# Softmax reciprocals widened by ScalarE and turned in whole transposes, and a reordered opening, in a fused attention and gated feed-forward kernel

## What is computed

```python
q_rot, k_rot = rotate(q), rotate(k)
scores = np.matmul(q_rot, k_rot.transpose(0, 1, 3, 2)) / sqrt(64)
attn = np.exp(scores - scores.max(axis=-1, keepdims=True))
attn = attn / (attn.sum(axis=-1, keepdims=True) + 1e-9)
x = np.matmul(attn, v)                       # to (2304, 512)
h = x @ w_in
g = np.maximum(h, 0) + alpha * np.minimum(h, 0)
out = g @ w_out
```

## Time and profile before

| | us |
|---|---|
| median of 3 runs (666.73 to 667.43) | 666.87 |
| the profiled execution | 668.44 |
| its span | 666.6 |
| PE busy in the span | 654.8 |
| DVE, ACT, POOL busy | 338.9, 320.5, 266.9 |
| attention, from the start to the first feed-forward matmul | 253 |

### The profile page before, as it was taken

How to read it: one execution, slowest core, us unless ns; L and a number is a source line. 1 busy time by engine, 2 the same in 40 slices (tenths; PEclk the granted TensorE clock), 3 DMA queues, 4 the chain that set the end, 5 groups by cost and what they waited for, 6 DMA issues and landing times.

```text
span 666.6 us, 14994 instructions
## 1 busy us (share of the span) xinstructions
PE 654.8 (98%) x5566; PEld 562.1 (84%) x5566; DVE 338.9 (51%) x779; ACT 320.5 (48%) x730; POOL 266.9 (40%) x254
## 2 busy tenths in 40 slices
PE   7899999999999999999999999999999999999998
PEld 6687778778877777988899999999999999999996
DVE  4677887878888773455523332333233323332222
ACT  2688888887888885333332223222322232223223
POOL 3755788888766223222222222222222222222222
PEclk8999999999999999999999999999999999999999
DMA  5596455544544436000010001000100010001001
GB/s 142 133 240 183 106 122 135 124 108 112 121 113 110 92 104 253 1 0 1 1 49 0 1 0 48 1 1 0 47 0 0 0 47 0 0 0 48 1 0 48
DMA packets 73309, 41.58 MB, mean 62 GB/s; under 512 B 59812, under 2 KB 64292, under 8 KB 72740
## 3 DMA queue, kind: packets, MB, share of 16 engines
q1 hardware_dynamic: 72978, 40.62, 23.3%
q10 hardware_dynamic: 274, 0.16, 0.1%
HBM read 22.95 MB, written 4.72 MB: 41 GB/s over the span
## 4 chain that ended last, share of the span: by engine, by line
PE 96%; DVE 1%; ACT 1%; DMA 1%; SPq 0%; issue 0%; POOL 0%; DVEq 0%
PE banks L772 30%; PE banks L801 30%; PE banks L713 9%; PE banks L607 8%; PE banks L687 5%; PE banks L636 3%; PE banks L709 3%; PE banks L581 2%; PE banks L658 2%; PE banks L663 1%; PE banks L562 1%; DMA cos_sb<-in_cos 1%; PE banks L589 1%; PE banks L666 0%; PE banks L654 0%
## 5 line engine op out<-in xcount | busy, mean ns | idle before, releaser
L529 POOL TENSOR_TENSOR g_lo<-g,g_hi 128x384 fp32r<-128x384 f32 (+1 forms) x98 | 99.7, 1018 | 306.9 <-ACT g_hi L959 303.7
L1123 DVE TENSOR_SCALAR g<-banks,alpha_sb 128x384 f32<-128x384 f32 (+1 forms) x98 | 59.7, 610 | 249.2 <-ACT pos L950 249.2
L772 PE MATMUL banks<-x_hi,w_in_lo 128*128 128x384 f32 x384 | 129.3, 337 | 0.0
L772 PE MATMUL banks<-x_hi,w_in_hi 128*128 128x384 f32 x384 | 129.2, 337 | 0.0
L772 PE MATMUL banks<-x_lo,w_in_hi 128*128 128x384 f32 x384 | 129.0, 336 | 0.0
L950 ACT ACTIVATE pos<-banks 128x384 f32<-128x384 f32 x96 | 47.2, 491 | 169.2 <-PE banks L772 169.2
L801 PE MATMUL banks<-w_out_hi,g_hi 128*128 128x512 f32 x288 | 114.9, 399 | 0.3
L801 PE MATMUL banks<-w_out_hi,g_lo 128*128 128x512 f32 x288 | 112.9, 392 | 0.0
L801 PE MATMUL banks<-w_out_lo,g_hi 128*128 128x512 f32 x288 | 111.9, 389 | 0.0
L959 ACT ACTIVATE g_hi<-g 128x384 fp32r<-128x384 f32 (+1 forms) x98 | 50.9, 519 | 116.5 <-DVE g L1126 116.5
L844 ACT ACTIVATE prob<-prob,nmax 128x576 f32<-128x576 f32 x128 | 98.3, 773 | 1.7 <-DVE prob L1014 1.7
(11 more groups left out here) (80 smaller groups left out, 920.4 us busy)
## 6 DMA issues: line engine op xcount, KB each, us to landing
q_swap<-q_nat SPq DMA_DIRECT2D x32, 256.0 KB, 3.6
k_swap<-k_nat SPq DMA_DIRECT2D x32, 144.0 KB, 3.1
out<-stage SPq DMA_DIRECT2D x18, 256.0 KB, 2.0
raw_q<-in_q SPq DMA_DIRECT2D x32, 128.0 KB, 2.8
raw_k<-in_k SPq DMA_DIRECT2D x32, 128.0 KB, 2.5
raw_v<-in_v SPq DMA_DIRECT2D x32, 128.0 KB, 2.3
w_in_raw<-in_moe_w_in SPq DMA_DIRECT2D x4, 1024.0 KB, 6.0
w_out_raw<-in_moe_w_out SPq DMA_DIRECT2D x8, 512.0 KB, 6.6
```

The costliest lines, as they stand in the source:

```text
L529: nc.gpsimd.tensor_tensor(g_lo[f % 2][:, part], g[f % 2][:, part], g_hi[f % 2][:, part].bitcast(F32), ALU.subtract).then_inc(g_lo_done, 1)
L772: mm = nc.tensor.matmul(h_ps[f % 2], w[:, j, cols], xx[:, j, :], start=(step == 0), stop=(step == 3 * CT - 1))
L1123: nc.vector.tensor_scalar(g[f % 2][:, part], h_ps[f % 2][:, part], 0.0, alpha_sb[:, f:f + 1], ALU.min, ALU.mult).then_inc(neg_done, 1)
```

## The change

The reciprocals: ACT widens them first (`widen`), copying each of the eight columns of the tiles 64 times into `inv_wide` (128 x 512, SBUF). PE then makes four whole 128 x 128 transposes of it in place of eight matmuls. DVE, no longer ACT, copies the 512 columns to `inv_sb`. The sums are kept in rows of three with a gap (`rsum` 3 x 4) and read as 3 x 3, the 1e-9 is an immediate of a `tensor_scalar` in place of a second operand, and the reciprocal follows at once.

The opening: ACT issues the keys and their remainders, SP the rest, so the cosines and the identity move up in SP's queue. U_MIXED is turned ahead of U_K in the work before pair 0, and in pair 0 it lies in the keys' bank pair (bank 2) in place of bank 1.

```diff
-OPENING_BANK = {U_Q: 2, U_K: 3, U_MIXED: 1}
+OPENING_BANK = {U_Q: 2, U_K: 3, U_MIXED: 2}
...
+        if u == U_K and isinstance(p, int) and p == 0:
+            return U_MIXED
...
-            rsum = sb(att, "rsum", [P, 2, TILES])
+            rsum = sb(att, "rsum", [P, 2, 3, 4])
+            sums = sb(att, "sums", [P, TILES])
...
-            load(0, 0)
+            heads(sp, 0, 0)
+            joined(sp, 0, 0)
             table(sp, cos_sb, cos, cos_in)
-            load(0, 1)
             sp.dma_start(ident[:, :], eye).then_inc(ident_in, 16)
...
             table(act, sin_sb, sin, sin_in)
+            joined(act, 0, 1)
+            heads(act, 0, 1)
...
-                if u != U_KQREM and has_prev(p):
+                if u == U_INV:
+                    pe.wait_ge(wide_done, p)
+                elif u == U_MIXED and has_prev(p):
                     pe.wait_ge(inv_done, p)
...
                     for i in range(QT):
-                        for r, n in zip(HEADS, (A_TILES[i], B_TILES[i])):
-                            mm = nc.tensor.matmul(bank[r, i * P:(i + 1) * P], inv[:, par, n:n + 1].to_broadcast([P, D]),
-                                                  ident[:, :], start=True, stop=True)
+                        mm = nc.tensor.transpose(bank[:, i * P:(i + 1) * P],
+                                                 inv_wide[:, i, :, :].rearrange("p h d -> p (h d)"), ident[:, :])
...
             turn(-1, -1, U_Q)
+            spread(-1, -1, U_MIXED)
             run_in(4)
             turn(-1, -1, U_K)
-            spread(-1, -1, U_MIXED)
             run_in(6)
...
+            def widen(p, t):
+                if not has_prev(p):
+                    return
+                act.wait_ge(inv_done, p)
+                if not (isinstance(p, int) and p == 1):
+                    act.wait_ge(turned, unit_count(p - 1, U_INV))
+                nc.scalar.activation(inv_wide[:, :, :, :], inv[:, (t - 1) % 2, 1:].rearrange("p (h i) -> p i h", h=2)
+                                     .unsqueeze(3).to_broadcast([P, QT, 2, D]), ACT.Copy).then_inc(wide_done, 1)
...
                 p = b * PAIRS + t
+                widen(p, t)
                 flat(p, U_QREM, t)
...
-                flat(p, U_INV, t)
                 flat(p, U_PA[0], t)
...
-                    nc.vector.tensor_tensor(rsum[:, par, :], rsum[:, par, :], tiny[:, :].to_broadcast([P, TILES]),
-                                            ALU.add).then_inc(sum_done, 1)
+                    nc.vector.tensor_scalar(sums[:, :], rsum[:, par, :, 0:3], 1e-9, None, ALU.add).then_inc(sum_done, 1)
...
-                    nc.vector.reciprocal(inv[:, par, :], rsum[:, par, :]).then_inc(inv_done, 1)
+                    nc.vector.reciprocal(inv[:, par, :], sums[:, :]).then_inc(inv_done, 1)
...
+                if h == 0:
+                    u = U_INV
+                    dve.wait_ge(turned, unit_count(p, u))
+                    nc.vector.tensor_copy(inv_sb[:, 0:QT * P], t_ps[bank_of(p, u)]).then_inc(evac[bank_of(p, u)], 1)
+                    dve.wait_ge(evac[bank_of(p, u)], evac_count(p, u))
                 dve.wait_ge(pv_done, n + 1)
...
                 reciprocals(p, t, 0)
+                reciprocals(p, t, 1)
                 flat(p, U_KQREM, t)
                 maxima(p, t, REM_TILE)
-                reciprocals(p, t, 1)
```

More of the change, by code:

```diff
@@ L95, in bank_of, with rank @@
         return OPENING_BANK.get(u, BANK_OF[u]) if isinstance(p, int) and p == 0 else BANK_OF[u]
+    def rank(p, u):
+        return U_Q + 0.5 if p < 0 and u == U_MIXED else u
     def tally(p, u, counted):
         if isinstance(p, int):
-            return sum(exists(r, w) for r in range(-1, p + 1) for w in counted if r < p or w <= u)
+            return sum(exists(r, w) for r in range(-1, p + 1) for w in counted
+                       if r < p or rank(p, w) <= rank(p, u))
         return p * len(counted) + (tally(PAIRS, u, counted) - PAIRS * len(counted))
@@ L194, in build @@
             raw_v = [sb(att, f"raw_v{i}", [P, ST, P]) for i in range(2)]
[L195 removed]
+            inv_wide = sb(att, "inv_wide", [P, QT, 2, D])
+            assert 2 * ST + QT >= CT * MT
             until_prob = used[0]
@@ L281, in build @@
         inv_done = sem("inv_done")
+        wide_done = sem("wide_done")
         pv_done = sem("pv_done")
@@ L340, in table, with heads, joined @@
             eng.dma_start(dst[:, QT, :], src[0:REM, QT, :].unsqueeze(0).to_broadcast([2, REM, D])).then_inc(landed, 16)
+        def heads(eng, p, side):
+            src, raw, landed = ((q_h, raw_q, q_in), (k_h, raw_k, k_in))[side]
+            for h in range(2):
+                eng.dma_start(raw[:, 0:QT, h * D:(h + 1) * D],
+                              src[p * 2 + h, 0:QT * P, :].rearrange("(t p) d -> p t d", p=P)).then_inc(landed, 16)
+        def joined(eng, p, side):
+            eng.dma_start(raw_q[side * REM:(side + 1) * REM, QT, :].rearrange("p (h d) -> p h d", h=2),
+                          (q_h, k_h)[side][bass.ds(p * 2, 2), QT * P:S, :].rearrange("h p d -> p h d")
+                          ).then_inc(q_in, 16)
         HEADS = (slice(0, D), slice(D, P))
@@ L358, in load @@
                     sp.wait_ge(rope_step, (p - 1) * 8 + side * 4 + 3)
-                for h in range(2):
-                    sp.dma_start(raw[:, 0:QT, h * D:(h + 1) * D],
-                                 src[p * 2 + h, 0:QT * P, :].rearrange("(t p) d -> p t d", p=P)).then_inc(landed, 16)
+                heads(sp, p, side)
                 if side == 0:
-                    for i, rems in enumerate((q_h, k_h)):
-                        sp.dma_start(raw_q[i * REM:(i + 1) * REM, QT, :].rearrange("p (h d) -> p h d", h=2),
-                                     rems[bass.ds(p * 2, 2), QT * P:S, :].rearrange("h p d -> p h d")).then_inc(landed, 16)
+                    for i in range(2):
+                        joined(sp, p, i)
             def swap(p, par, side):
@@ L646, in spread @@
                 elif u != U_INV and has_next(p):
-                    turned_in(p, 1)
-                if u != U_KQREM and has_prev(p):
+                    turned_in(p, 0 if isinstance(p, int) and p < 0 else 1)
+                if u == U_INV:
+                    pe.wait_ge(wide_done, p)
+                elif u == U_MIXED and has_prev(p):
                     pe.wait_ge(inv_done, p)
@@ L881, in flat @@
                     jobs = [(pt_half(t % 2, u), half_bank(bank))]
-                else:
-                    if not (isinstance(p, int) and p == 1):
-                        act.wait_ge(x_done, (p - 1) * 2)
-                    jobs = [(inv_sb[:, 0:QT * P], bank)]
                 for dst, src in jobs:
@@ L972, in _ @@
             table(act, sin_sb, sin, sin_in)
+            joined(act, 0, 1)
+            heads(act, 0, 1)
             act.wait_ge(padded, 2)
             nc.scalar.activation(prob_rem[REM:P, 0:1], raw_v[0][REM:P, QT, 0:1], ACT.Exp)
-            for u in OF_NEW:
-                hi(-1, u, -1)
+            hi(-1, U_Q, -1)
+            hi(-1, U_MIXED, -1)
+            hi(-1, U_K, -1)
             def batch(b):
@@ L1084, in normalise @@
                 n = (p - 1) * 2 + h
+                if h == 0:
[3 more added lines that the diff above has]
+                    dve.wait_ge(evac[bank_of(p, u)], evac_count(p, u))
                 dve.wait_ge(pv_done, n + 1)
-                if h == 0:
-                    dve.wait_ge(evac[bank_of(p, U_INV)], evac_count(p, U_INV))
                 half = slice(h * HALF, (h + 1) * HALF)
@@ L1190, in _ @@
                 nc.vector.tensor_tensor(rot4, rot4, halves, ALU.add).then_inc(first_step, 1)
-            for u in OF_NEW:
-                lo(-1, u, -1)
+            lo(-1, U_Q, -1)
+            lo(-1, U_MIXED, -1)
+            lo(-1, U_K, -1)
             def batch(b):
```

6 lines of the change are left out of this document (2 added, 4 removed).

## The result

The kernel takes 656.6 us after the change (median of 4 runs, 656.47 to 656.79) against 666.8 before (4 runs, 665.85 to 667.43): a ratio of 0.9849, 95% interval 0.9835 to 0.9863. It is faster by 10.2 us; forecast were 7.8, and the time lies 2.5 us under the 659.1 of the forecast, inside its range. The profiled execution after took 656.47 us.

A forecast was written before the change was run, and what follows sets the result against it. PE was taken to bound attention, busy 40.00 of 40 us, ACT next at 86%. Reciprocals 5.8 plus opening 2.0 made 7.8 us: profiled execution 660.6, median 659.1, range 653.8 to 663.0.

The forecast's parts named there:

- The reciprocals on PE: Middle of each period: four whole transposes replace eight matmuls, 1.03 us becomes 0.67, saving 0.36 us 16 times, 5.8 us.
- 4 x 0.125 + 0.17 = 0.67: PE's time in us for the reciprocals: four whole transposes at 0.125 each plus 0.17 for the change of tiling.
- Rival 1: Reciprocals on PE: each whole transpose costs only a pair of small ones, 0.068 us; 11.4 us saved, median 655.5; 30%.
- Is another engine late: Every period: DVE's extra copy and ACT's `widen` hold up no PE work, the new sum taking 0.17 us; cost nothing.
- Rival 3: Head of the period: the sum still waits for POOL in ten periods, `widen` is late; 3.5 us back, 662.6; 10%.
- The copy on DVE: Middle of the period: DVE copies the 512 turned columns in 0.68 us; costs nothing, at worst 0.2 us a period.
- The opening: Work up to period 1: 0.6 + 0.6 + 1.0 - 0.25 = 2.0 us saved.
- The cosines' 0.6 us: First loads: with the keys' remainders issued by ACT, the cosines and everything behind come earlier; 0.6 us, bounds 0 and 0.77.
- U_MIXED ahead of the keys: Before the first scores: U_MIXED moves into PE's wait for the rotated keys, saving 0.6 us (12.44 - 11.82).
- The bank: Pair 0: with U_MIXED in bank 2 its first transposes don't wait for DVE's last read; 1.0 us saved.
- The -0.25 for a late `widen` in period 1: Period 1: `widen` would end at 33.2, after the 32.92 at which U_QREM's copy starts today; 0.25 us lost.
- The clock: Opening: shorter PE idle stretches may shorten the second half-clock spell; nothing counted in the sum, 1.6 us kept for the range.

The follow-up runs named there:

- e8: The changed kernel with each of the four whole transposes of the reciprocals made twice: 663.87 us, ratio 0.9962 to the kernel before.
- e7: The changed kernel with plain float32 matmuls with `ident` in place of the four whole transposes: 664.42 us, ratio 0.9974 to the kernel before.
- e1: The changed kernel with the old opening (loads, order and bank as before), so the reciprocals' part alone: 658.79 us, ratio 0.9889 to the kernel before.
- e6: The changed kernel with the sum made from two SBUF inputs again, 1e-9 coming from a tile: 664.84 us, ratio 0.9986 to the kernel before.
- e9: The changed kernel with the copy of the turned reciprocals back on ACT in place of DVE: 657.11 us, ratio 0.987 to the kernel before.
- e3: The changed kernel with all first loads on SP's queue in the old order: 656.75 us, ratio 0.985 to the kernel before.
- e10: The changed kernel with the U_MIXED of the work before pair 0 behind the keys again: 657.07 us, ratio 0.9865 to the kernel before.
- e4: The changed kernel with U_MIXED of pair 0 back in bank 1: 658.95 us, ratio 0.9895 to the kernel before.
- e5: The changed kernel with the reciprocal behind the remainder maximum again, `widen` kept: 676.9 us, ratio 1.0157 to the kernel before.
- e12: The changed kernel with the first three loads of w_in one period later on SP's queue: 656.82 us, ratio 0.986 to the kernel before.
- e13: The kernel before with the opening's edits alone, the first U_MIXED no longer waiting for the keys: 664.2 us, ratio 0.9969 to the kernel before.

## Why the prediction was right, point by point

**The bound** was read rightly. e8 puts 7 us of transposes on PE's list, and PE's time is what the kernel pays.

**The reciprocals on PE**: forecast 0.36 us a period, measured 1.03 - 0.59 = 0.44. The term "4 x 0.125 + 0.17 = 0.67" was mis-sized in its 0.125, which is 0.105 to 0.108. What I took from the idle matmul was right in kind (one record for a transpose, two for a matmul) and a sixth too long in size: its pair of records and the change of tiling, 0.42 us, were read from one place in the opening, and e7's eight records behind one another give (1.09 - 0.17) / 8 = 0.115; the rest is that a transpose's record costs a little less than a matmul's. Rival 1 (0.068) was twice as far off on the other side: 0.44 us where 0.59 was measured and 0.67 forecast. Its 655.5 lies nearer to the measured time all the same, because 1.6 us of clock came on top; the time alone would have pointed to the wrong price. The rule of the Trainium skill ("TensorE: Matmul & The Clock Gate", Terms) that transpose mode is four times faster for FP32 does not hold for these: e7 and after give 0.23 against 0.105, 2.2 times. Their weight loads last 0.14 us each and may set that pace; no run tells. Nor do the 275 ns that the Trainium skill gives for a 128x128 transpose inside a kernel ("TensorE: Matmul & The Clock Gate", Part 4, beside a figure for bf16) stand for the price in a row of transposes: the length of one record is near it here (272 to 329 ns), and they start 0.105 us apart.

In fifteen periods that is 6.6 us. In the last one less was gained: from these reciprocals to the block's next matmuls it was 3.43 us before (262.99 to 266.42) and is 3.17 after (251.35 to 254.52), 0.26. Together 6.9 us. The average period fell by 0.48, not 0.44, but that is the first one, which before began at half clock; the other fourteen fell by 0.44, just PE's saving. At equal clock e1 measured 6.8 for what I had put at 5.8.

**Is another engine late**: the forecast of 0.17 us for the new sum held in all sixteen periods, and e6 shows what it is worth, 8 us (662.8 against 654.75 at clock 1.000). It is no gain over before, whose sum waited without PE feeling it; it is what the new order would lose. Rival 3 had that loss at 3.5 us, by `widen` alone. The sum now starts 0.33 us behind POOL's instruction, not 0.75 (99.13 and 98.80; 106.18 and 105.43 before), so it would wait 1.18 us, not 0.75, and DVE's copy of U_KQREM behind the reciprocal is late as well. The account of `widen` (it "just fits") held too: ACT's copies start right behind it, at the moment PE would have let them. I had them wait for PE still; they wait for `widen`, without PE feeling it, so that sign of the prediction failed and its sum held. The rule of the Trainium skill ("VectorE: DVE Perf Modes", What auto-detection actually checks) that 3 and 9 as outermost counts keep the op from the two-port mode agrees with 156 to 166 ns in all sixteen, of which 12 start under a running POOL instruction.

**The copy on DVE** costs nothing, and e9 shows that it could have stayed.

**The opening** came out near its sum (2.0 forecast; 1.85 at clock 1.000, by one execution of e1) with wrong items, and that is luck. The cosines' 0.6 us failed: I had two bounds, 0 if the transfers bind and 0.77, and took the upper end because SP's issue stood late. It was 0.08, and e3 shows 0. U_MIXED ahead of the keys was 0.6 in the forecast and 0 to 0.5 in e10: the 0.6 was read at half clock, and at full clock U_MIXED takes 0.37 us (9.46 to 9.83). The bank was 1.0 and is 0.9 to 1.45 in e4: besides the 1.19 us also the 1.33 and 0.29 of waiting behind it went, and a new 1.27 us came in front of the second transposes. I had written that these "aren't held"; they are. The -0.25 for a late `widen` in period 1 didn't come: behind 27.85 the trace lists no wait of PE in that period. The first scores start at 13.20 where I had 13.8, but 1.13 us of their 1.83 is clock, which the sum had at nothing.

**The clock** was left out of the sum, kept for the range as up to 1.6 us in the second stretch. It is the 1.6 us between 8.6 at equal clock and 10.2 between medians, 0.5 of it by which four executions of before were taken; and it is not only the second stretch. That it came out at just the 1.6 of the range is chance. Of 60 executions of the eight kernels that have all of the opening's edits (after, e5 to e9, e12, e13), 33 have a mean clock of 1.000 and none one of 0.992; of before's 57 it is 5 and 12.

So 659.1 became 656.6 by +1.0 for the reciprocals, -0.15 for the opening and +1.6 for the clock.

## What to carry to other kernels

When a step is moved, its wait moves with it: with the old one, U_MIXED ahead of the keys cost 3.4 us that its own wait gives back. A step put at the head of an engine's idle time is free only as long as what feeds it is early; here 0.17 us instead of 0.75 for nine numbers, and a reciprocal two instructions up, were each worth more than the matmuls saved (8 and 20 us against 7). What such a delay costs is read from everything that stands behind it in the engine's list, not only from the one consumer that one has in mind. Between executions that differ in granted clock, compare spans at equal mean clock, or the parts of a change won't add up.

## What the runs showed of the hardware that I had not expected

- How long PE stands still in the opening doesn't by itself tell what the clock does. In after it was 2.52 us up to 9.07, and the clock stayed at 1.00; in e5, whose opening is the same, it was 1.76 us up to 9.16, and the clock was 0.73 in the window from 9.5 to 10 and 0.50 from 10 to 13. What else decides stays open.
- That DVE's instruction with two inputs from SBUF ends with POOL's was expected. How long 128x9 elements can take by it was not: 1.18 us in e6 and up to 1.31 in e13, against 0.165.
- ACT widens 128x8 numbers to 128x512 by a broadcast source in 0.63 us, as long as a plain copy of 512 columns.
